# Recurrence and MLP turns interleaved on one core: turns 0 and 1 in another order

## The reference

```python
# attention with decay, over 4 x 8 sequences of 768 steps, head size 48
y[t]  = r[t] @ (state + (u * k[t]) outer v[t])
state = w[t][:, None] * state + k[t] outer v[t]
# MLP on 3072 tokens: 384 -> 2048 -> 384
h = x @ w_in;  g = h * tanh(softplus(h));  x2 = g @ w_out
# routing: tokens take experts in order of all logits, 384 places in each of 8 experts
logits = x2 @ w_gate
# experts, 384 -> 1024 -> 384
out[mask] = relu(x2[mask] @ w1[e]) @ w2[e]
```

## Time and profile before

| | us |
|---|---|
| median of 3 runs | 801.81 (801.06 to 802.01) |
| the profiled execution | 799.13 |
| its span, first to last instruction | 797.4 |
| TensorE busy in the span | 770.9 |
| VectorE busy | 624.8 |
| ScalarE busy | 425.1 |
| GpSimd busy | 293.3 |

### The profile page before, as it was taken

One profiled execution on the slowest core, in us unless ns is written; L12 is line 12 of the kernel. 1 busy time (PEld: TensorE's weight loads), 2 busy tenths in 40 slices (PEclk: granted clock), 3 DMA queues, 4 the chain that ended last, 5 costly groups with the idle time before them and its releaser, 6 DMA issues.

```text
span 797.4 us, 17084 instructions
## 1 busy us (share of the span) xinstructions
PE 770.9 (97%) x6784; PEld 578.0 (72%) x6784; DVE 624.8 (78%) x1075; ACT 425.1 (53%) x703; POOL 293.3 (37%) x244
## 2 busy tenths in 40 slices
PE   8899999999999999999999999997999999999994
PEld 8888878787878787878787877555565565666662
DVE  8968999999998999998999965867776767766220
ACT  2478759595968595868686779500121221222221
POOL 4424482627272727263636350001221231222311
PEclk9999999999999999999999999995999999999998
DMA  9962256463656464655464365105424415415500
GB/s 308 376 208 65 77 198 235 151 234 143 233 190 212 152 226 160 210 213 197 172 199 185 111 216 191 61 21 189 169 89 152 188 61 189 186 44 208 218 31 30
DMA packets 47791, 133.49 MB, mean 167 GB/s; under 512 B 5344, under 2 KB 19808, under 8 KB 45664
## 3 DMA queue, kind: packets, MB, share of 16 engines
q1 hardware_dynamic: 38880, 93.07, 33.6%
q0 software_dynamic: 5376, 34.61, 11.8%
q10 hardware_dynamic: 3456, 4.72, 1.7%
HBM read 97.78 MB, written 34.60 MB: 166 GB/s over the span
## 4 chain that ended last, share of the span: by engine, by line
PE 82%; DVE 11%; ACT 2%; issue 2%; DMA 2%; POOL 0%; SPq 0%; ACTq 0%; DVEq 0%
PE bank L425 79%; DVE cmp L1285 2%; PE bank L708 1%; DMA stage<-in_moe_w_out 1%; DVE g_lo L1385 1%; ACT t_sb L785 1%; PE bank L450 1%; PE bank L511 1%; DVE inv L987 1%; DMA k_tok<-in_k 1%; DVE t_sb L1364 1%; DVE rdec L1002 0%; DVE t_sb L1357 0%; DVE t_sb L1360 0%; DVE tmp L1275 0%
## 5 line engine op out<-in xcount | busy, mean ns | idle before, releaser
L425 PE MATMUL bank<-x_hi,win_hi 128*128 128x256 f16 x576 | 158.4, 275 | 2.3 <-DVE x_lo L1050 1.4
L425 PE MATMUL bank<-x_lo,win_hi 128*128 128x256 f16 x576 | 158.2, 275 | 0.0
L425 PE MATMUL bank<-x_hi,win_lo 128*128 128x256 f16 x576 | 158.0, 274 | 0.0
L1514 POOL TENSOR_TENSOR g_lo<-t_sb,g_hi 128x512 f16<-128x512 f32 x88 | 122.2, 1421 | 46.7 <-ACT g_hi L785 46.7
L425 PE MATMUL bank<-wout_hi,g_hi 128*128 128x392 f16 (+1 forms) x416 | 129.1, 317 | 0.8 <-issue 0.8
L425 PE MATMUL bank<-wout_lo,g_hi 128*128 128x392 f16 (+1 forms) x416 | 128.8, 316 | 0.0
L425 PE MATMUL bank<-wout_hi,g_lo 128*128 128x392 f16 (+1 forms) x416 | 128.7, 316 | 0.0
L785 ACT ACTIVATE g_lo<-bank 128x384 f16<-128x384 f32 x64 | 31.4, 490 | 143.4 <-PE bank L425 143.4
L1498 POOL TENSOR_TENSOR dv<-v_tok,dot 128x384 f32<-128x384 f32 x24 | 29.8, 1241 | 187.8 <-DVE dot L1017 187.8
L785 ACT ACTIVATE g_hi<-t_sb 128x512 f16<-128x512 f32 x96 | 56.5, 623 | 54.6 <-PE bank L425 54.4
L1066 DVE TENSOR_TENSOR t_sb<-t_sb,h_sb 128x512 f32<-128x512 f32 x96 | 83.0, 912 | 2.0 <-ACT t_sb L785 1.4
(11 more groups left out here) (183 smaller groups left out, 1592.3 us busy)
## 6 DMA issues: line engine op xcount, KB each, us to landing
stage<-in_moe_w SPq DMA_DIRECT2D x22, 768.0 KB, 6.3
w_split<-stage SPq DMA_DIRECT2D x22, 768.0 KB, 4.5
fold_w<-in_moe_w SPq DMA_DIRECT2D x10, 768.0 KB, 9.0
w_split<-fold_w SPq DMA_DIRECT2D x10, 768.0 KB, 7.7
wt<-in_w_turned SPq DMA_DIRECT2D x24, 258.0 KB, 3.3
kt<-in_k_turned SPq DMA_DIRECT2D x24, 256.0 KB, 2.6
rt<-in_r_turned SPq DMA_DIRECT2D x24, 256.0 KB, 2.8
r_tok<-in_r SPq DMA_DIRECT2D x24, 192.0 KB, 6.0
```

The lines of the kernel that those rows point to most:

```text
L425: return nc.tensor.matmul(*a, **k)
L1514: G.tensor_tensor(g_lo[:, j * GW:(j + 1) * GW], t_sb[:, j * GW:(j + 1) * GW], g_hi[:, j * GW:(j + 1) * GW], ALU.subtract).then_inc(s["glo" ...
```

## The change

In turn 0 the first two tiles are made in halves, one chunk of 128 tokens each, and the halves of chunk 0 stand ahead of the wait for chunk 1. The first halves of turn 1's tiles 0 to 2 are made in turn 0 between the steps of chunk 3, the second halves after its `turn_x`. The fold is no longer made in rows of 12 but one product behind every third product of nine tiles or half tiles. The values of chunks 2 and 3 stand singly behind tile products.

The gate products of turn 0 move from a row of their own to places between the h copies of turn 1; each is followed by its rounding (ScalarE) and its remainder (GpSimd) in the slots of turn 1. The copy of h(1, j) waits for `gated(0, j)`. Chunk 5's scores come two slots later, its values in sum 4, its transposes after sum 5; on VectorE its masks come after four of the gate products of turn 1 and after the splits of pieces 6 and 7. At the end, the load of the function table moves behind the copies of the last logits; the maximum, picks and one-hot of the first 20 columns of tokens are made in turn 11, those of the last 4 after it; constants of the routing move from turn 11 to turn 10.

```diff
+            FOLDS = {(0, 4): 6, (0, 5): 6, (0, 7): 6, (1, 0, 0): 6, (1, 0, 1): 4, (1, 1, 1): 4, (1, 2, 1): 4, (1, 3): 6,
+                     (1, 4): 6}
...
                     for t, (a, b) in enumerate(ops):
                         last = mm(hb[HB[j]][:, f * TOK:(f + 1) * TOK], a, b, start=t == 0, stop=t == len(ops) - 1)
+                        if t % 3 == 1 and 3 * f + t // 3 < folds:
+                            fold_one()
...
             def turn(i, slot):
                 n0, n1 = CH * (i + 1), CH * (i + 1) + 1
-                between = {6: (n0, 0, 12), 7: (n0, 12, 16), 10: (n1, 0, 12), 11: (n1, 12, 16)}
-                here = between.get(slot, ()) if 1 <= i < NI - 1 else ()
-                if slot < NJ:
+                late = 2 if i == 1 else 0
+                between = {6: (n0, 0, 12), 7: (n0, 12, 16), 10 + late: (n1, 0, 12), 11 + late: (n1, 12, 16)}
+                if i == 0:
+                    between = {6: (n0, 0, 16)}
+                here = between.get(slot, ()) if i < NI - 1 else ()
+                if (i, slot) in ((0, 0), (0, 1), (1, 0), (1, 1), (1, 2)):
+                    half_tile(i, slot, 1)
+                elif slot < NJ:
                     tile(i, slot, *here)
                 elif i >= 1:
                     sums(i - 1, slot - NJ, slice(0, None), *here)
                 if i == 0:
                     if slot == 3:
-                        folded([0])
                         scores(2)
                     elif slot == 5:
                         keys(2)
-                        values(2)
                     elif slot == 6:
                         turn_x(2)
+                    elif slot == 7:
                         scores(3)
-                    elif slot == 7:
+                        half_tile(1, 0, 0)
                         keys(3)
-                        values(3)
+                        half_tile(1, 1, 0, 3, 0, 12)
+                        half_tile(1, 2, 0, 3, 12, 16)
                         turn_x(3)
-                        folded([1])
...
-            warm(ident[:, :], 5)
+            half_tile(0, 0, 0)
+            half_tile(0, 1, 0)
```

On ScalarE:

```diff
                 if slot < NJ:
+                    if i == 1:
+                        rounded(0, slot)
                     copied(i, slot)
                     if slot >= 1:
                         arctan(i, slot - 1)
                     tanh(i, slot)
...
+                    if i == 1 and slot == 14:
+                        turn_x(n1)
                     rounded(i, slot - NJ - 1)
...
-                        if i == NI - 1:
-                            nc.scalar.preload_act_table_set("sigmoid_and_others")
...
             finish(NI - 1, 1)
+            nc.scalar.preload_act_table_set("sigmoid_and_others")
```

On VectorE, turn 1 has a list of its own (lines left out are of the same kind), and the picks take a range of columns:

```diff
                 dve.wait_ge(s["h"], NJ * i + j + 1)
+                if i == 1:
+                    dve.wait_ge(s["g"], j + 1)
...
+                elif slot == 8:
+                    low_x(4)
+                    inverse(5, 1)
+                    key_side(5)
+                    query_side(5)
+                elif slot == 9:
+                    gated(1, 0)
+                    gated(1, 1)
+                    split_piece(6)
+                elif slot == 10:
+                    gated(1, 2)
+                    gated(1, 3)
+                    split_piece(7)
+                elif slot == 11:
+                    masks(5)
+                    dots(5)
+                    gated(1, 4)
...
+                    if i == NI - 1:
+                        dve.wait_ge(s["L"], OLD)
+                        link(V.tensor_reduce(L[:, NT * E:NT * E + 1], L[:, 0:OLD * E], AX.X, ALU.max,
+                                             apply_absolute_value=True))
+                        pick_expert(slice(0, OLD))
+                        one_hot_expert(slice(0, OLD))
...
-            V.tensor_reduce(amax[:, :], L[:, :], AX.X, ALU.max, apply_absolute_value=True).then_inc(s["maxin"], 1)
-            pick_expert()
-            one_hot_expert()
+            V.tensor_reduce(amax[:, :], L[:, OLD * E:NT * E + 1], AX.X, ALU.max, apply_absolute_value=True
+                            ).then_inc(s["maxin"], 1)
+            pick_expert(slice(OLD, NT))
+            one_hot_expert(slice(OLD, NT))
```

More of the change, by code:

```diff
@@ L513, in turn_x, with fold_one @@
                 last.then_inc(s["xT"], 1)
+            FOLDS = {(0, 4): 6, (0, 5): 6, (0, 7): 6, (1, 0, 0): 6, (1, 0, 1): 4, (1, 1, 1): 4, (1, 2, 1): 4, (1, 3): 6,
+                     (1, 4): 6}
+            to_fold = [(t, k3) for t in range(FT) for k3 in range(KT)]
+            def fold_one():
+                t, k3 = to_fold.pop(0)
+                q, f = t // (FT // 4), t % (FT // 4)
+                last = mm(ab[0][:, t * E:(t + 1) * E], wot[q][:, k3, f * P:(f + 1) * P], w_gate[:, k3, :],
+                          start=k3 == 0, stop=k3 == KT - 1)
+                if f == FT // 4 - 1 and k3 == KT - 1:
+                    last.then_inc(s["fold"], 1)
             def tile(i, j, values_of=None, begin=0, end_at=0):
@@ L869, in turn @@
                             split_piece(7)
-                        elif slot == 7:
-                            keys(3)
-                            turn_x(3)
                 elif slot == NJ:
@@ L883, in turn @@
                         nc.scalar.preload_act_table_set("sigmoid_and_others")
-                else:
+                elif i >= 1:
+                    if i == 1 and slot == 14:
+                        turn_x(n1)
                     rounded(i, slot - NJ - 1)
-                    if slot == 12 and with_att:
+                    if i == 1 and slot == 12:
+                        keys(n1)
+                    if slot == 12 and with_att and i > 1:
                         turn_x(n1)
@@ new lines, in one_hot_expert, with second_turn @@
+            def one_hot_expert(js=slice(0, NT)):
+                hot = V.tensor_tensor(oh[:, js, :], over_j(eighths[:, :], js.stop - js.start), over_e(pick[:, js]),
+                                      ALU.is_equal)
+                if js.stop == NT:
+                    hot.then_inc(s["oh"], 1)
+            def second_turn(slot):
+                if slot == 0:
+                    copied(1, 0)
+                    gated(0, 1)
+                    inverse(4, 1)
+                    key_side(4)
+                    query_side(4)
+                elif slot == 2:
+                    gated(0, 2)
+                    copied(1, 2)
+                    gated(0, 3)
+                elif slot == 3:
+                    masks(4)
+                elif slot == 4:
+                    gated(0, 4)
+                    copied(1, 4)
+                    gated(0, 5)
+                    dots(4)
+                elif slot == 5:
+                    gated(0, 6)
+                    gated(0, 7)
+                    products(5)
+                elif slot == 6:
+                    dve.wait_ge(s["foldhi"], 1)
+                    V.scalar_tensor_tensor(wout_lo[:, :, DM:DE],
+                                           ab[0][:, 0:FT * E].rearrange("p (f e) -> p f e", e=E), SW_GATE,
+                                           wout_hi[:, :, DM:DE], ALU.mult, ALU.subtract).then_inc(s["foldlo"], 1)
+                    copied(1, 6)
+                    sum_x(4)
+                    inverse(5, 0)
+                elif slot == 7:
+                    new_state(4)
+                    split_piece(5)
+                elif slot == 8:
[15 more added lines that the diff above has]
+                    gated(1, 4)
+                elif slot == 12:
+                    gated(1, 5)
+                    gated(1, 6)
+                elif slot == 13:
+                    sum_x(5)
+                    gated(1, 7)
+                    new_state(5)
+                    products(6)
+                elif slot == 14:
+                    low_x(5)
+                    inverse(6, 0)
+                elif slot == 15:
+                    inverse(6, 1)
+                    key_side(6)
+                    query_side(6)
@@ L1097, in turn @@
                         dots(2)
+                        split_piece(4)
                     elif slot == 6:
@@ L1527, in turn @@
                         own(n1)
+                elif i == 0:
+                    if slot == 8:
+                        diagonal(4)
+                        remainder(0, 0)
+                elif i == 1 and slot < 12:
+                    if slot == 5:
+                        own(4)
+                    elif slot == 6:
+                        diagonal(5)
+                    if 1 <= slot < NJ:
+                        remainder(0, slot)
+                    elif slot > NJ:
+                        remainder(1, slot - NJ - 1)
+                elif i == 1:
+                    if slot == 12:
+                        own(5)
+                    remainder(1, slot - NJ - 1)
+                    if slot == SLOTS - 1:
+                        remainder(1, NJ - 1)
                 elif slot == 0 and with_att:
```

162 lines of the change are left out of this document (91 added, 71 removed).

## The result

The changed kernel takes 805.31 us (median of 11 runs, 804.19 to 810.19), the kernel before in the same session 801.58 (798.78 to 803.13): ratio 1.0050, 95% interval 1.0036 to 1.0064. It is slower by half a per cent, where 800.8 was forecast. The profiled execution took 805.36 with a span of 803.6. TensorE is busy 767.7 us of it (before 770.9), and the span is 6.2 longer: the products did get cheaper, and the waits got dearer.

What follows compares the result with a forecast made beforehand. TensorE was taken to set the pace, with VectorE almost as busy in turn 1. Turn 2's start +1.0 and the tail -2.0 gave -1.0, so 798.1 profiled and 800.8 median; own range 799 to 803, 8 in 10 within 795.2 to 804.3.

Steps and rivals of the forecast that it cites:

- The tail: End of the kernel: table load moved and steps on 4 token columns bring the first count 2.0 us earlier (1.2 to 2.4).
- Half tiles: Tiles of turns 0 and 1 made in halves: 0.055 us a product of 128 columns, 1.0 us a half tile.
- rival 3: Half tiles at 0.081 us a product: +1.4 in the chain to 63.6, total 802.2; chance 0.08.
- the fold's gain: Turns 0 and 1: single fold products cut 10.7 to 5.8 us, -4.9, spent in TensorE's tile 7 wait for keys(4).
- VectorE's queue from low_x(4) to the end of the masks: Turn 1: inverse, kdiv, rdec, four gate products, two splits and chunk 5's masks run from 90.1 to 100.5.
- the first rounding copy starts at 67.3: ScalarE, after turn 0's chain ends at 63.6: first rounding copy at 67.3 instead of 69.84, 2.5 us gained.
- the missed 4.8: Start of turn 2 on TensorE: forecast at 112.6, +1.0 to before; it came at 117.41, +5.8.
- the second wait: Turn 0, ahead of tile 4: TensorE idles 1.8 us for ScalarE's copy of 39.1; tile 4 starts at 39.2.
- the round trip of 2.6: Turn 1, ScalarE and GpSimd: rounding, remainder and tanh take 0.76 + 1.3 + 0.55 us a tile; six end at 83.0.
- the three signs of being wrong: Round trip not 2.6 us; VectorE's queue from low_x(4) to masks not 10.3; tail steps on 4 columns costing as on 24.
- Rival 2: Clock: waits before tile 4 and sum 4 each cost two slow stretches, another 1.7 us each, total 804.2; chance 0.22.
- Rival 1: Products set the pace: masks before 97.5 or no clock fall at 39, turn 2 at 107.5, total 795.7; chance 0.25.

Runs made afterwards that it cites:

- the fold-alone run: Kernel before with the fold's 48 products standing singly in tiles 4 to 7 of turn 0 and 0 to 3 of turn 1: 803.48 us, ratio 1.0029.
- the last version: Changed kernel with splits of pieces 5, 6, 7 moved out of turn 1, idle products around scores(2) and ten ahead of the half tile: 796.60 us, ratio 0.9941.
- the reordered versions: Changed kernel with chunk 5's masks early on VectorE: 805.58 us, ratio 1.0068; with all chunk 5 work ahead of most gate products: 811.77 us, ratio 1.0100.
- the splits moved: Kernel before with the tail edits and VectorE's splits of w_out pieces 4 to 7 moved out of turn 1: 800.80 us, ratio 0.9997.
- the rows of eight: Changed kernel with turn 0's gate products, roundings and remainders in rows of eight again, as in the kernel before: 809.76 us, ratio 1.0099.

## Why the prediction was wrong

**Right, by its steps.** The tail: -2.0 forecast, -2.1 in the profile. Half tiles: 0.055 a product between 68.25 and 68.31, and rival 3 falls. The Trainium skill (TensorE: Matmul & The Clock Gate, Back-to-back issue gap) has 81 ns for this size in a stream with weight loads; here the trace does not agree, and the measurement decides.
TensorE's timeline, changed kernel, a half tile with folds:

```profile
68.25 0.22 PE L425 MATMUL bank<-x_hi,win_hi 128*128 128x128 f16 x1
68.31 0.22 PE L425 MATMUL bank<-x_lo,win_hi 128*128 128x128 f16 x1
68.36 0.34 PE L425 MATMUL bank<-w_gate,fold_w 128*128 128x8 f32 x2
68.56 0.22 PE L425 MATMUL bank<-x_hi,win_lo 128*128 128x128 f16 x1
```

The last wait of TensorE, ahead of sum 4 for the masks, forecast 3.6, is 3.47. Scores(2) at 36.52 (36.3). That the fold's gain is spent in waiting: the fold-alone run shows it. VectorE's queue from low_x(4) to the end of the masks, forecast 10.4, took 10.50 (94.97 to 105.47), and from sum 4's first value product to turn 2, with the 1.7 for the clock in it, 12.0 were forecast and 11.89 came. The mechanism was the forecast's own; what failed are the sizes of the steps ahead of low_x(4).

**The step that failed first** is "the first rounding copy starts at 67.3". It started at 70.30, and this 3.0 is most of the missed 4.8. Its parts: the w_out piece came 1.3 later than in the trace before (38.46, and the prediction kept the old 37.18), so the second wait was 2.96 and not 1.8, and tile 4 began at 40.64 and not 39.2, 1.4 late. Tiles 4 and 5 took 7.6 us where 6.6 stood in the sum, 1.0 more: a tile with six folds takes 2.80 at the higher level (53.84 to 56.64) and not 2.7, and the low clock cost 2.0 and not 1.2. The remaining 0.5 are the pieces behind, of which the single folds are measured: 0.14 in a full tile (45.23 to 45.37), 0.195 in a half tile (68.36 to 68.56), where 0.12 was charged (between half tiles up to 0.05 more). Undoing the only edit of VectorE's order ahead of the w_out piece did not bring it back to 37.18. It need not have been the change: the other four profiles with this part of turn 0 as before have the split at 37.62 to 38.25. The prediction rested on the earliest of them.

**The step that failed second** is the round trip of 2.6. From the first rounding to low_x(4) 22.8 us were forecast and 24.67 came. The six round trips took 17.2 us and not 15.7, 2.87 each, because the remainders took 1.49 on average and not 1.3. The other 0.4 are between the last of them and low_x(4). So of the three signs of being wrong that the prediction named, the round trip's is the one that came.

3.0 + 1.9 = 4.9, and the two steps behind, both right to 0.1, give the 0.1 back: 4.8.

**The rivals.** Rival 2, the clock, named a right cause and part of the size. Its sign came (tile 5 ended at 48.28, and it said 46.8 or later). The place around scores(2) did bring 6.8 us at the lower level, though TensorE was idle for a third of them, so that it cost 0.8 more than was charged and not 1.7; the place ahead of sum 4 brought only 3.4. That its 804.2 is near the measured 805.31 is in good part luck. It left out the third place, the wait of 1.26 ahead of the second half tile, which had been costed at nothing; in some executions 10.2 us at the lower level follow, and by their mean clock (0.968) the two near 810 are of this kind. Neither of them was profiled; ten idle products in that wait took the slower executions away in the last version (of which there are five), and in the changed kernel took the two near 810 away but left two slower ones of low clock. Rival 1, the products set the pace, needed the masks before 97.5 and a clock that does not fall. The last version comes near to this: masks from 97.22 to 98.50, no fall, turn 2 at 109.86 where the rival said 107.5, and it measures 0.9941 of the time before (797.1 on the 801.81 shown then) where that rival said 795.7. TensorE still waits 1.43 and 0.85 us in its turn 1.

**What the shift consists of.** In the changed kernel turn 2 stands at 117.41; without the falls at 113.91; with VectorE's splits moved out as well at 109.86. So of the way down to the last version 3.5 are the clock's and 4.05 are VectorE's list, each from a pair of single traces. That it is the list's content and not its order is what the reordered versions suggest, though falls of the clock disturb their medians: the wait went from the masks to x_tok and from there to x_lo of chunk 5. In the kernel before both engines were near full in turn 1. There less work for TensorE alone gave nothing (the fold taken apart), and less work for VectorE alone gave nothing (the splits moved, with the loss in turn 0 told above); with TensorE's part made cheaper by the change, moving VectorE's splits paid. The prediction saw both shares and priced VectorE's queue, but took what stands in it as given.

**What stays open**: why the clock stays low for 3.4 us behind one wait and for 6.8 or 10.2 behind another; why executions of one kernel differ in it; what the wait near 550 is; where that part of the 3.4 us comes from which the products around scores(2) gave beyond the clock's 2; and what part half tiles alone have, which was not run.

## What to carry to other kernels

When two engines are both near full in a stage, making one's work cheaper can buy a wait, as the fold alone did here, and the wait can buy a fall of the clock: price the fall, and look for work of the second engine that can move to a stage where it idles, before reordering it. Where the wait can't be removed, idle products in it are worth trying: 38 of them around scores(2) took the changed kernel from 1.0050 to 1.0008 of the time before. Count a fall only where the engine works: of 6.8 us at the lower level that began inside a wait, 2.2 were lost. And take the start of a chain that hangs on a DMA from more than one trace: the same piece came at 37.2 to 38.6 us over the profiles here.

## What the runs showed of the hardware

In the changed kernel's profile the granted clock was low for 3.4 us behind the wait of 3.47 at 105.52, for 6.8 from inside the wait of 2.96 on, and not at all behind the wait of 1.26 at 67.89; other profiles have 6.8 us behind the same wait of 3.48 (the rows of eight) and 10.2 behind the same wait of 1.26. The second trace of the kernel before has a fall of 3.4 us at 65.5 with no wait of TensorE over 0.1 us in the 8 us ahead of it. So the length of a wait does not tell the cost; a forecast should carry nothing and 5.1 us as bounds for a wait like these. At the lower level a single fold product between half-tile products took about 0.40 us instead of 0.195 (67.80 to 68.20 in the run with moved splits and products around scores(2)):

```profile
67.80 0.54 PE L425 MATMUL bank<-w_gate,fold_w 128*128 128x8 f32 x2
68.20 0.27 PE L425 MATMUL bank<-x_hi,win_lo 128*128 128x128 f16 x1
```
